# A fused attention and feed-forward kernel on one core: five transfers placed later in the SyncE queue

## The reference

```python
p_packed = sm_attn(p, k, v)                 # (8, 8, 32, 64)
x = sm_attn(q, p_packed, p_packed)          # (8, 8, 576, 64) -> 4608 x 512
xn = x / sqrt(mean(x * x) + 1e-6) * rms_g
x = (silu(xn @ w_gate) * (xn @ w_val)) @ w_out      # 512 -> 1536 -> 512
out = ((x @ w1) * (x @ w2) @ w3) @ w_out2           # 512 -> 1024 -> 512
```

## Time and profile before

| | us |
|---|---|
| median of 3 executions | 1361.45 (1361.1 to 1361.8) |
| the profiled execution, its own time | 1361.45 |
| its span, first to last instruction | 1359.7 |
| PE busy | 1349.2 |
| DVE, ACT, POOL busy | 827.3, 425.2, 127.8 |

### The profile page before, as it was taken

One profiled execution on the slowest core, in us unless ns is written; L12 is line 12 of the kernel. 1 busy time (PEld: TensorE's weight loads), 2 busy tenths in 40 slices (PEclk: granted clock), 3 DMA queues, 4 the chain that ended last, 5 costly groups with the idle time before them and its releaser, 6 DMA issues.

```text
span 1359.7 us, 24236 instructions
## 1 busy us (share of the span) xinstructions
PE 1349.2 (99%) x9992; PEld 1163.3 (86%) x9992; DVE 827.3 (61%) x1488; ACT 425.2 (31%) x836; POOL 127.8 (9%) x117
## 2 busy tenths in 40 slices
PE   9999999999999999999999999999999999999998
PEld 7677788887878888878888899999999999999997
DVE  4667666576665755766654668655656464656544
ACT  4353533434334334343333423221212121221211
POOL 0201001001010010100100531010101010110100
PEclk9999999999999999999999999999999999999999
DMA  9783454533635426341435350202021020202001
GB/s 327 240 278 95 126 158 140 174 108 85 203 114 169 139 83 193 98 131 48 138 104 204 127 182 1 63 0 63 1 63 51 13 63 1 63 1 63 1 32 31
DMA packets 89870, 141.84 MB, mean 104 GB/s; under 512 B 30624, under 2 KB 40864, under 8 KB 87968
## 3 DMA queue, kind: packets, MB, share of 16 engines
q1 hardware_dynamic: 63648, 133.99, 30.7%
q10 hardware_dynamic: 26112, 6.30, 2.1%
HBM read 112.99 MB, written 27.28 MB: 103 GB/s over the span
## 4 chain that ended last, share of the span: by engine, by line
PE 97%; DVE 2%; DMA 0%; ACT 0%; issue 0%; SPq 0%; DVEq 0%
PE psum L769 9%; PE psum L768 9%; PE psum L767 9%; PE psum L688 8%; PE psum L689 7%; PE psum L690 7%; PE psum L709 6%; PE psum L710 6%; PE psum L708 6%; PE psum L789 5%; PE psum L790 5%; PE psum L791 5%; PE psum L652 4%; PE psum L636 1%; PE psum L615 1%; PE psum L668 1%
## 5 line engine op out<-in xcount | busy, mean ns | idle before, releaser
L769 PE MATMUL psum<-xo_hi,w_lo 128*128 128x256 f32 x1008 | 285.3, 283 | 0.0
L768 PE MATMUL psum<-xo_lo,w_hi 128*128 128x256 f32 x1008 | 285.2, 283 | 0.0
L767 PE MATMUL psum<-xo_hi,w_hi 128*128 128x256 f32 x1008 | 285.1, 283 | 0.0
L688 PE MATMUL psum<-a_hi,m_hi 128*128 128x288 f32 x768 | 239.8, 312 | 0.2 <-DVE g_s L1240 0.2
L689 PE MATMUL psum<-a_lo,m_hi 128*128 128x288 f32 x768 | 226.6, 295 | 0.0
L690 PE MATMUL psum<-a_hi,m_lo 128*128 128x288 f32 x768 | 226.1, 294 | 0.0
L768 PEld LDWEIGHTS psum<-xo_lo,w_hi 128*128 128x128 f32 x1008 | 193.4, 192 | 1.4
L767 PEld LDWEIGHTS psum<-xo_hi,w_hi 128*128 128x128 f32 x1008 | 193.4, 192 | 1.4
L769 PEld LDWEIGHTS psum<-xo_hi,w_lo 128*128 128x128 f32 x1008 | 193.4, 192 | 0.0
L688 PEld LDWEIGHTS psum<-a_hi,m_hi 128*128 128x128 f32 x768 | 144.3, 188 | 54.4 <-issue 46.2
L1240 DVE SCALAR_TENSOR_TENSOR g_s<-g_s,psum 128x288 f32<-128x288 f32 x192 | 86.3, 450 | 114.9 <-ACT g_s L1005 113.9
(11 more groups left out here) (144 smaller groups left out, 1882.2 us busy)
## 6 DMA issues: line engine op xcount, KB each, us to landing
w_in<-in_w_gate SPq DMA_DIRECT2D x24, 1024.0 KB, 5.4
w_in<-in_w_val SPq DMA_DIRECT2D x24, 1024.0 KB, 5.5
kT<-in_kT SPq DMA_DIRECT2D x8, 1152.0 KB, 11.1
v_sb<-in_v SPq DMA_DIRECT2D x8, 1152.0 KB, 7.4
qT<-in_qT SPq DMA_DIRECT2D x16, 576.0 KB, 4.0
y_scratch<-g_res SPq DMA_DIRECT2D x9, 1024.0 KB, 8.7
x<-y_scratch SPq DMA_DIRECT2D x32, 256.0 KB, 5.6
out<-b_res SPq DMA_DIRECT2D x8, 1024.0 KB, 5.3
```

The lines of the kernel that those rows point to most:

```text
L688: nc.tensor.matmul(in_ps[which], hi, a2_hi[:, t, par, :], start=par == 0, stop=False)
L767: nc.tensor.matmul(dst, hi, xo_hi[:, i, c, :], start=c == 0, stop=False)
L768: nc.tensor.matmul(dst, hi, xo_lo[:, i, c, :], start=False, stop=False)
L769: last = nc.tensor.matmul(dst, lo, xo_hi[:, i, c, :], start=False, stop=c == 1)
```

## The change

Five of the transfers that SP issues around the change from the first stage to the second are placed later in its queue. Nothing is added or left out, and no wait of a transfer is changed. All five stood ahead of the wait for `fuse_done` and now stand behind it: the pieces 2 and 3 of `w_in`, both halves of the queries of batch 1, and the values of batch 1.

```diff
             load_kp(1)
-            load_v(1)
             store_wf(0)
-            load_w_in(0, 2)
             spread_r(0)
-            load_w_in(0, 3)
-            load_q(1, 0)
-            load_q(1, 1)

             sp.wait_ge(fuse_done, 2 * 4)
             load_wo(0)
+            for part in range(2, 4):
+                load_w_in(0, part)
             load_wo(1)
             store_wf(1)
+            load_q(1, 0)
             sp.wait_ge(wf_stored[1], 16)
             load_wo(2)
+            load_v(1)
             load_wo(3)
+            load_q(1, 1)
```

## The result

| | before | after |
|---|---|---|
| median of 4 executions, us | 1361.28 (1360.65 to 1361.80) | 1371.63 (1370.39 to 1372.65) |
| ratio | | 1.0076, 95% interval 1.0058 to 1.0093 |
| the profiled execution, its own time | 1361.45 | 1372.39 |
| its span | 1359.7 | 1370.6 |

What follows compares the result with a forecast made beforehand. PE was taken as the bound, busy for 1349.2 of 1359.7 us. The terms 2.2 - 0.3 + 1.7 = 3.6 us on top of 1361.45 gave 1365.1 us, with a range from 1362.9 to 1367.2.

Steps and rivals of the forecast that it cites:

- Views and bound: Whole kernel: PE busy 1349.2 of 1359.7 us; from 60 to 110 us PE waits on no transfer.
- Part 1: Early place of the values, at 29 us: nothing waits there, so moving them is worth 0, at most 0.2 us.
- Part 2: Piece 2 of `w_in`, issued behind wo 0, lands at 73.45 us; PE idles 2.2 us ahead of `M` 0,2.
- Part 3: Piece 3 lands 2.6 us later, at 76.1; `M` 0,3 does not wait for it and loses its 0.30 us on DVE.
- Part 4: Wo 1 lands at 78.0 us, moving ACT's split of row 1 by 1.9 us; cost to PE in slot 4: 0.
- Part 5: Values behind the stored second half and wo 2 land at 91.0 us; PE idles another 1.7 us ahead of `PV` 1,0.
- Part 6: Queries of batch 1, next pieces of `w_in`, wo 2 and wo 3 land before they are read: all 0.
- Rival C: PE's clock falls in one of the waits, for 4 us, losing 2 us: 1367.1; chance 0.05.
- A: Only `M` 0,2 is late, the values are not held up by wo 2; delay 1.9 us: 1363.35; chance 0.17.
- B: Not slower: piece 2 lands by 71.3 us and the values before 87.4, time 1361.4; chance 0.05.
- D: Transfers share the queue instead of following each other; delay about 4.5 us: 1366; chance 0.10.
- Sum: Total delay of PE from the waits at `M` 0,2 and `PV` 1,0: 2.2 - 0.3 + 1.7 = 3.6 us.

## Why the prediction was wrong

*Views and bound.* Right: PE was the bound, no moved transfer was late before, and what was put ahead of PE reached the end.

*Part 1, the values leave their early place.* Right, nothing up to 66 us gained or lost by it.

*Part 2, `M` 0,2.* Right in size: a wait of 2.2 forecast, 2.18 measured. Piece 2 took 6.7 us from issue, 66.73 to 73.45 was the forecast. The row of wo 1 in the same place was the right one to scale.

*Part 3, `M` 0,3.* Right that PE does not wait there and the 0.3 us go. Wrong that the piece follows after 2.6 us. The transfers issued at 65.7, 66.2 and 66.8 in the changed kernel are piece 3, wo 1 and the store (us to landing):

```profile
w_in<-in_w_val SPq DMA_DIRECT2D x1, 1024.0 KB, 10.5
...
wo_raw<-in_w_o SPq DMA_DIRECT2D x1, 768.0 KB, 11.9
...
wf_scratch<-wf_second SPq DMA_DIRECT2D x1, 1024.0 KB, 13.8
```

Piece 3 landed 4.3 us behind piece 2, at 76.2, because from 72 to 76 us the queue moved about 300 GB/s and not the 406 of the earlier trace rows:

```profile
72.00:74.00 2.00, 1.94 (x23) 1.13 (x24) 1.08 (x2) 0.75 (x1) 0.00 (x0) 1.00 1.01 296
74.00:76.00 2.00, 2.00 (x14) 1.73 (x12) 1.67 (x3) 1.33 (x4) 0.00 (x0) 1.00 0.97 315
```

The same dip is in the profiles of all nine kernels in which piece 3 follows piece 2 directly (a window of 236 to 296 GB/s between 72 and 76 us). What causes it was not tried and stays open. The store landed 15.8 us after wo 0 was issued instead of the 14.3 forecast.

*Part 4, wo 1.* The landing was 1.6 us later with the rest, ACT stood 2.8 us before the split of row 1, and PE waited 0.7 at `AT`. As the prediction said, the wait at the values swallowed it.

*Part 5, the values.* Right mechanism, mis-sized term: 3.4 us of wait against 1.7. 1.5 us of the difference are the dip above. Another 0.8 is the load itself, 5.6 us behind wo 2 where I took 4.8: the upper bound, 5.5 from 215 GB/s, was the true one, and the one worked out from the time to landing was not. `AT`'s 0.7 stands on the other side.

*Part 6, "all 0": the step that failed.* It looked at when each moved transfer is read, and at the next pieces of `w_in`. It did not look at what else is behind them in the same DMA engines: the keys and values of batch 2, and with them ACT's store, which has a reader too, since ACT must have its landing before it writes `g_hx` again. In the kernel before that store was issued at 91.38 and took 7.4 us, so it landed at 98.8, and ACT wrote `g_hx` again at 102.2: 3.4 us of room. Behind ACT PE had 1.9 us more (4.65 us of ACT's wait became 2.76 of PE's). I worked out neither. Measured: 2.8 us of PE and a fall of the clock. First in, first out held for SP's queue; between SP's queue and ACT's the engines took turns. The run with the values alone moved and the keys and values of batch 2 late shows the mechanism by taking it away, with all of the 3.7 us.

*Rival C, the clock.* I gave it 5 in 100 because the one idle stretch that I looked at, at the end, was over 4 us long when the clock fell. One row with a long wait says nothing of shorter ones. In the profiles the clock fell behind waits of 1.9, 2.1, 2.2, 2.3, 2.4, 2.8, 3.4 and 4.3 us, and did not fall behind others of 1.8, 2.2, 2.4, 2.4, 2.5 and 3.1. That is 8 of 14, and each fall was worth up to 1.7 us. So the 5 in 100 was the second step that failed: with waits of 2.2 and 1.7 us in the forecast a fall had to be priced at about even odds.

*Rivals A, B, D.* None came. B had been the case of the fit of the Trainium skill ("DMA: Bandwidth & Descriptors", section "Anatomy of one DMA — SWDGE (gpsimd) path"), with 4.4 us for 1 MB; piece 2 took 6.7 with 0.25 MB ahead of it.

*Sum.* 3.6 forecast. The wait for the values was 1.7 too small, the store in slot 10 was missed with 2.8, the clock with 3.4, and `AT` with 0.7: 12.2 in the profiled execution, of which the earlier start of the clock hides 1.5.

## What to carry to other kernels

When transfers move behind a wait, don't stop at the reader of each moved transfer. List everything that is queued behind them, on the other engines' queues too, until the backlog is gone, and for each ask who waits for its landing; the smallest store can be the one that decides. Look at the size of the packets that it will meet, not only at the bytes: here a load in rows of 12 KB cost each small packet beside it 0.8 us. Price each new idle stretch of PE of two us and more with a possible fall of its clock on top, and look in the profile of before for how much slack a landing has, not only for whether anyone waits.

## What the runs showed of the hardware

- A store of 64 KB issued by ACT landed 14.3, 13.8, 7.4 or 4.8 us after its issue, depending on what SP had queued before it. It did not wait for all of it: the one issued at 84.58 in the changed kernel landed at 93.4, ahead of three transfers that SP had issued sooner (they landed at 94.9, 96.2 and 99.0). The Trainium skill, "DMA: Bandwidth & Descriptors", section "Queues, rings and completion order", says that each DMA engine takes turns between the queues that have work, a packet at a time. The trace of the changed kernel agrees, with 79 packets of SP's queue and 78 of ACT's from 103.5 to 107.5 us. The turns did not help the store there, because each of SP's packets took 0.8 us, and its own first packet moved only 3.7 us after its issue.
- The clock of PE fell to half behind 8 of 14 waits of 1.8 to 4.3 us, at a price of up to 1.7 us each time. Matmuls in place of the wait, whose results nobody reads, kept it up in the three profiles in which they were tried, behind the wait that they filled. That they make the kernel faster is not clear of the noise (medians 1368.84 and 1366.28, intervals that overlap).
- Executions of the same kernel differ by 3 to 5 us (1359.2 to 1362.6 over 24 of the kernel before, 1360.0 to 1363.9 over 19 on another chip, 1361.6 to 1366.75 over ten with the pieces of `w_in` back in their early places). In the two profiles shown matmuls of 512 columns went from 0.63 to 0.39 us some 10 and some 7 us into the span, which is 1.5 us of it.
- In the changed kernel 2 MB of weights queued back to back moved at 296 to 315 GB/s in their second half, and at 277 to 348 with `w_in` alone moved, against 406 with a store behind a load.
